# Attention and two MLPs on one core: another order of the first loads, and weights split up to two tiles sooner

## The chip, the cores and the metric

The kernel runs on one core of a Trainium2 chip. Its engines are TensorE (PE; PEld is its weight load), VectorE (DVE), ScalarE (ACT), GpSimd (POOL) and SyncE (SP), which here issues all the transfers; the core's 16 DMA engines carry them. The metric is the device time of one execution in microseconds (us); lower is better.

## The reference, cut to what matters

```python
def _attn_ref(q, k, v):                      # 2 x 8 heads, 768 positions, head size 64
    k_sum = k.reshape(B, H, nb, 32, D).max(axis=3)       # one summary key per block of 32
    v_sum = v.reshape(B, H, nb, 32, D).mean(axis=3)
    scores_l = scale * q @ k^T, kept where |i - j| < 16
    scores_s = scale * q @ k_sum^T + log(32)
    a = softmax(concat(scores_l, scores_s))
    return a @ concat(v, v_sum)

def _moe_ref(x, w_in, w_out, alpha):         # 1536 tokens, 512 -> 2048 -> 512
    h = x @ w_in
    return (max(h, 0) + alpha * min(h, 0)) @ w_out

def _moe2_ref(x, w_in, w_out, a, b):
    h = x @ w_in
    P = a[0] + a[1]*h + a[2]*h*h + a[3]*h*h*h
    Q = 1 + |b[0]|*|h| + |b[1]|*h*h
    return (P / (Q + 1e-6)) @ w_out

reference: _moe2_ref(_moe_ref(_attn_ref(q, k, v)))
```

All of it is float32.

## The kernel before

The 1536 tokens are cut into four chunks of 384 (two per batch entry). Attention is cut into 16 jobs: a job is one chunk and one pair of heads, and a chunk's four jobs give the four 128-row tiles of its `x`. Jobs 0 to 3 (the first chunk) run alone at the start; the jobs of each later chunk are woven into the steps of the first MLP on the chunk ahead of it. An MLP step (`i`, with chunk `c` and tile `f`) takes one of 16 tiles of 128 hidden columns: `hidden1(i)` is 12 matmuls into a bank `hid`, the activation is done on DVE (L810, L812), and `output1(i)` is 12 matmuls into the four banks `acc`, two steps later. The second MLP follows in the same manner with `hidden2` and `output2`.

The stages of a job are KQ (transposes of keys and queries), KX (transposes of the other keys), SC (scores, their maxima on DVE and exponentials on ACT), NM (probabilities, DVE), TR (transposes of the probabilities; ACT copies them into `pt`), AV and SU (block means of the values), and PV (probabilities times values; ACT and DVE split the result into `x_hi` and `x_lo`). Products are made of three matmuls with high and low parts, so every weight tile is split before use: ACT writes `w_in_hi` and `w_out_hi` (`w_in_high`, `w_out_high`, both through the copy at L541), POOL subtracts them from the raw tile to get `w_in_lo` (L505) and `w_out_lo` (L510). Raw weights come two tiles at a time: `load_w_in(0, n)` and `load_w_out(0, n)` bring tiles 2n and 2n+1, and `load_w(0, n)` does both.

Every engine goes through its own list in order, and waits on semaphores. For the first chunk the lists of PE, ACT and DVE are written out by hand (`FIRST_PE`, `FIRST_ACT`, `FIRST_DVE`, L69 to L78). In `FIRST_ACT` the split of `w_in` tile 0 stands ahead of (2, TR), (3, SC), (1, PV), (3, SU) and (3, TR). In `FIRST_PE` (3, AV) stands ahead of (1, PV), (2, PV) and (3, TR), and the first products `hidden1(0)` behind (3, TR). (3, AV) waits for the sums that POOL makes (L472) of the values that `first_rest(3)` loads.

In the loop over steps ACT does at each step, in this order: the attention stages that belong to the step, then `weights(0, f + 3)` (both splits of one tile, L663 to L667), then `g1_high(i)`, the high part of the activated tile, whose low part DVE makes (`g1_low`, L787). `hidden1(i)` waits for the low part of step i-2, whose bank it takes. Job 4 has its KQ at step 0, SC at step 2, TR at the start and PV at the end of step 3; job 5 has its KQ at step 4.

SP's list is the order of the loads (L370 to L416). It has waits of its own: `load_keys(j)` for j > 4 waits until PE has done the key transposes of job j-1 (`pe_k`), since `k_raw` has a single buffer, and then for the query transposes (`pe_q`); in `load_values` the copies at L342 wait for `pool_v0`. While SP waits, nothing behind it in its list is issued.

Of the kernel before, what the change touches and what calls it, by code (L numbers as in the profile page):

```python
# [13 lines left out]
def attention_two_mlps(nc, q, k, v, w_in1, w_out1, alpha, w_in2, w_out2, a_coef, b_coef, out):  # L14
# [17 lines left out]
    KD, FT = DM // P, DF // P  # L32
# [123 lines left out]
    with ExitStack() as ctx:  # L156
# [53 lines left out]
        def half(j):  # L210
            return chunk(j) % 2

        def batch(j):
            return chunk(j) // 2

        def pair(j):
            return j % NPAIR
# [13 lines left out]
        def kx_jobs(j):  # L231

            return sum(1 for n in range(j + 1) if half(n) == 0)

        def heads(p):

            return slice(2 * p, 2 * p + 2)
# [12 lines left out]
        def vgroup(j):  # L250
            return pair(j) // 2
# [12 lines left out]
        def _(sp):  # L264
            def load_pair(dst, rows, src, loaded):

                for h in range(2):
                    sp.dma_start(dst[0:rows, :, h, :], src[h].rearrange("(t p) d -> p t d", p=rows)).then_inc(loaded, 16)  # L268

            def first_k(p):  # L270
                hs = heads(p)
                load_pair(k_raw0[:, :, hs, :], KROWS[0], k[0, hs, 0:4 * KROWS[0], :], k0_loaded[p])

            def first_q(p):
                hs = heads(p)
                load_pair(q_raw0[:, :, hs, :], P, q[0, hs, 0:CH, :], q0_loaded[p])

            def first_kx(p):
                hs = heads(p)
                load_pair(kx_raw0[:, :, hs, :], KXROWS, k[0, hs, 4 * KROWS[0]:S, :], kx0_loaded[p])  # L280

            def load_keys(j):
                b, hs, n = batch(j), heads(pair(j)), KROWS[half(j)]
                s0 = 0 if half(j) == 0 else CH - WINDOW
                if j > NPAIR:
                    sp.wait_ge(pe_k, j)
                load_pair(k_raw, n, k[b, hs, s0:s0 + 4 * n, :], k_loaded)
                if j > NPAIR:
                    sp.wait_ge(pe_q, j)
                load_pair(q_raw, P, q[b, hs, half(j) * CH:half(j) * CH + CH, :], q_loaded)  # L290
                if half(j) == 0:
                    if kx_jobs(j) > NPAIR + 1:
                        sp.wait_ge(pe_kx, kx_jobs(j) - 1)
                    load_pair(kx_raw, KXROWS, k[b, hs, 4 * KROWS[0]:S, :], kx_loaded)
# [3 lines left out]
            def edge(half):  # L298

                n = KW - WINDOW  # L300
                if half == 0:
                    return 0, slice(WINDOW, KW), slice(0, n), slice(0, WINDOW)
                return UNITS - 1, slice(0, n), slice(S - n, S), slice(n, KW)

            def windows_of(b, h, half):

                rows = v[b, h]
                first = QT - WINDOW if half == 0 else CH - WINDOW
                return bass.AP(rows.tensor, rows.offset + first * D, [[D, KW], [QT * D, UNITS - 1], [1, D]])

            def first_edges():
                t, rows, inside, outside = edge(0)
                sp.dma_start(vw0[rows, t, :, :], v[0, :, inside, :].rearrange("h p d -> p h d")).then_inc(edges0_loaded, 16)
                sp.dma_start(vw0[outside, t, :, :], v[0, :, 0:WINDOW, :].rearrange("h p d -> p h d")).then_inc(edges0_loaded, 16)

            def first_rest(p):
                hs = heads(p)
                sp.dma_start(v_all[p][0:RP, :, :], v[0, hs, :, :].rearrange("h (p t) d -> p h (t d)", t=RT)).then_inc(rest0_loaded[p], 16)

            def first_windows(p):  # L320
                for h in range(2 * p, 2 * p + 2):
                    sp.dma_start(vw0[0:KW, 1:UNITS, h, :], windows_of(0, h, 0)).then_inc(v0_loaded[p], 16)

            def load_values(j):
                b, h0, s = batch(j), 2 * pair(j), j % 2
                if j >= NPAIR + 2:
                    sp.wait_ge(pe_v, j - 1)
                t0, t1 = (1, UNITS) if half(j) == 0 else (0, UNITS - 1)
                for h in range(2):
                    sp.dma_start(vw[0:KW, s, t0:t1, h, :], windows_of(b, h0 + h, half(j))).then_inc(v_loaded[s], 16)  # L330
                t, rows, inside, outside = edge(half(j))
                sp.dma_start(vw[rows, s, t, :, :], v[b, h0:h0 + 2, inside, :].rearrange("h p d -> p h d")).then_inc(v_loaded[s], 16)
                sp.dma_start(vw[outside, s, t, :, :], v[b, h0:h0 + 2, 0:WINDOW, :].rearrange("h p d -> p h d")).then_inc(v_loaded[s], 16)
                if batch(j) == 0:
                    sp.wait_ge(pool_v0, 1)
                else:
                    sp.wait_ge(pool_vs, vgroup(j) + 1)
                for h in range(2):
                    r = (pair(j) % 2) * 2 * NB + h * NB
                    rows = vsum0[:, pair(j), h, :] if batch(j) == 0 else vsum[r:r + NB, vgroup(j), :]  # L340
                    src = rows.unsqueeze(1).broadcast_to([NB, UNITS, D])
                    sp.dma_start(vw[KW:KU, s, :, h, :], src).then_inc(v_loaded[s], 16)  # L342
# [9 lines left out]
            def load_w_in(m, n):  # L352

                if m:
                    sp.wait_ge(pe_h, LAST + WG * (n + 1))
                for f in range(WG * n, WG * (n + 1)):
                    sp.dma_start(w_in_raw[:, f, :, :], w_in_v[m][:, f, :, :]).then_inc(w_in_loaded[n], 16)

            def load_w_out(m, n):

                if m:
                    sp.wait_ge(pe_o, LAST + WG * (n + 1))
                fs = slice(WG * n, WG * (n + 1))
                sp.dma_start(w_out_raw[:, fs, :], w_out_v[m][:, fs, :]).then_inc(w_out_loaded[n], 16)

            def load_w(m, n):
                load_w_in(m, n)
                load_w_out(m, n)
# [3 lines left out]
            first_kx(0)  # L372
            first_k(1)
            first_q(1)
            first_kx(1)
            first_rest(0)
            first_k(2)
            first_q(2)
            first_kx(2)
            first_rest(1)  # L380
            first_k(3)
            first_q(3)
            first_rest(2)
            first_kx(3)
            first_windows(0)
            first_edges()
            first_rest(3)
            first_windows(1)
            sp.dma_start(alpha_rows[0:FT, :], alpha.rearrange("(f p) -> f p", p=P)).then_inc(alpha_loaded, 16)
            load_w_in(0, 0)  # L390
            first_windows(2)
            first_windows(3)
            load_w_out(0, 0)
# [1 line left out]
            load_keys(4)  # L395
            load_w_out(0, 1)
            load_w(0, 2)
            load_w(0, 3)
            load_values(4)
            load_w(0, 4)  # L400
            load_keys(5)
            load_w(0, 5)
            load_values(5)
            load_w(0, 6)
# [134 lines left out]
        def _(act):  # L539
# [55 lines left out]
            def w_in_high(m, f):  # L595
                act.wait_ge(w_in_loaded[f // WG], 16 * WG * (m + 1))
                if m == 0 and f == 3:
                    act.wait_ge(pool_v0, 1)
                copy(w_in_hi[f][:, :, :].rearrange("p k c -> p (k c)"), w_in_raw[:, f, :, :].rearrange("p k c -> p (k c)")).then_inc(act_w_in, 1)
# [5 lines left out]
            def weights(m, f):  # L605
                w_in_high(m, f)
                w_out_high(m, f)
# [41 lines left out]
            for i in range(STEPS):  # L649
                c, f = i // FT, i % FT  # L650
                if i == FT + FT // 2:
                    act.wait_ge(consts_loaded, 32)
                    act.activation(ab[:, 4:6], ab[:, 4:6], ACT.Abs).then_inc(act_ab, 1)
                    act.wait_ge(act_ab, 1)
                slot(c + 1, f, 0)
                if i < R1:
                    g1_high(i)
                if i >= FT and f == LAG1 - 1:
                    chunk_done(c - 1, (0, 1))
                slot(c + 1, f, 1)  # L660
                if i >= FT and f == LAG1 - 1:
                    chunk_done(c - 1, (2, 3))
                slot(c + 1, f, 2)  # L663
                if c == 0:

                    if f + 3 < FT:
                        weights(0, f + 3)  # L667
                if i >= LAST + LW:
                    weights(1, i - LAST - LW)
                if i >= R1:  # L670
                    act.wait_ge(pe_o, i - R1 + 1)
                    g1_high(i)
# [8 lines left out]
            for i in range(STEPS + 2):  # L681
                n, f = i // FT, i % FT
# [404 lines left out]
```

## Time and profile before

| | |
|---|---|
| Median of 3 runs | 622.32 us (622.29 to 622.75) |
| The profiled execution's own time | 622.29 us |
| Its span in the profile | 620.6 us, so 1.7 us lie outside the span |
| PE busy over the span | 605.1 us, 98% |
| ACT, DVE, POOL busy over the span | 312.0, 414.3, 197.1 us |
| Share of PE in the chain that ended last | 93% |

The page gives busy time, which hides where an engine of 98% has its other 2%. So the rows below are of the first 60 us for the most part, where PE and the DMA engines change places as the one that the others wait for. Starts are us from the span's start. In a row of the timeline, what stands in brackets is how long the engine had been idle ahead of the instruction and what released it; a duration of a merged row covers all of its instructions. The granted clock of TensorE (PEclk) is 1.00 at full speed.

### The profile page before, as it was taken

Reading aid. Unit: us, or ns where it says so; the run is one execution under the profiler, and the core shown is the slowest. Engines: PE = TensorE matmul, PEld = TensorE weight load, DVE = VectorE, ACT = ScalarE, POOL = GpSimd, SP = SyncE. Lnnn points to the kernel's source line nnn. Section 1 sums busy time; section 2 is a strip of 40 time slices with the busy share of each in tenths; the row PEclk is TensorE's granted clock in tenths of the full one; section 3 lists DMA queues with packets and bytes.
Section 4 is the critical chain, followed back from the end, with each engine's and each line's share of the span. In section 5 each row is a group of like instructions: output and inputs, shape, how many; then the busy total and the mean of one; then the engine's idle time right before and its main releaser. Section 6 shows DMA issues by size and latency. Waiting matters only on the chain.

```text
span 620.6 us, 10573 instructions
## 1 busy us (share of the span) xinstructions
PE 605.1 (98%) x3897; PEld 563.5 (91%) x3897; DVE 414.3 (67%) x953; ACT 312.0 (50%) x778; POOL 197.1 (32%) x221
## 2 busy tenths in 40 slices
PE   5799999999999999999999999999999999999997
PEld 4689999999999999999999899899899899999996
DVE  4665555555654555455555699778978788778775
ACT  4784644333332433232434587657755765656564
POOL 4564559000000000000333375334434434433431
PEclk9899999999999999999999999999999999999999
DMA  8999606311222022001344300001000000001001
GB/s 181 225 265 262 165 7 132 68 28 36 64 51 45 6 50 51 2 1 62 110 135 137 102 1 1 1 0 53 1 1 1 34 18 1 0 2 51 1 2 51
DMA packets 79539, 37.30 MB, mean 60 GB/s; under 512 B 56496, under 2 KB 72896, under 8 KB 79296
## 3 DMA queue, kind: packets, MB, share of 16 engines
q1 hardware_dynamic: 79488, 36.63, 23.2%
q8 instruction: 31, 0.51, 0.3%
q14 instruction: 20, 0.16, 0.1%
HBM read 32.58 MB, written 3.15 MB: 58 GB/s over the span
## 4 chain that ended last, share of the span: by engine, by line
PE 93%; SPq 3%; DVE 1%; DMA 1%; issue 1%; ACT 0%
PE acc L947 15%; PE acc L949 14%; PE acc L948 14%; PE hid L947 11%; PE hid L949 11%; PE hid L948 11%; PE att L947 4%; PE att L949 4%; PE att L948 4%; SPq L268 2%; PE att L937 2%; PE att L874 2%; PE att L909 2%; PE att L916 1%; DMA w_in_raw<-in_moe_w_in_dram 1%
## 5 line engine op out<-in xcount | busy, mean ns | idle before, releaser
L947 PE MATMUL hid<-x_hi,w_in_hi 128*128 128x384 f32 x384 | 130.2, 339 | 0.0
L949 PE MATMUL hid<-x_hi,w_in_lo 128*128 128x384 f32 x384 | 129.1, 336 | 0.0
L948 PE MATMUL hid<-x_lo,w_in_hi 128*128 128x384 f32 x384 | 128.9, 336 | 0.0
L510 POOL TENSOR_TENSOR w_out_lo<-w_out_raw,w_out_hi 128x512 fp32r<-128x512 f32 x32 | 41.3, 1294 | 219.4 <-ACT w_out_hi L541 219.2
L947 PE MATMUL acc<-g_hi,w_out_hi 128*128 128x384 f32 x256 | 91.1, 356 | 0.0
L531 POOL TENSOR_SCALAR qpart<-habs,ab 128x384 f32<-128x384 f32 x64 | 44.0, 688 | 143.1 <-ACT poly L689 142.5
L949 PE MATMUL acc<-g_hi,w_out_lo 128*128 128x384 f32 x256 | 86.8, 339 | 0.0
L948 PE MATMUL acc<-g_lo,w_out_hi 128*128 128x384 f32 x256 | 86.5, 338 | 0.0
L541 ACT ACTIVATE g_hi<-hid 128x384 fp32r<-128x384 f32 x96 | 48.4, 504 | 67.8 <-PE acc L949 59.9
L787 DVE TENSOR_TENSOR g_lo<-hid,g_hi 128x384 fp32r<-128x384 f32 x64 | 35.6, 556 | 65.2 <-ACT g_hi L541 65.2
L949 PE MATMUL acc<-w_out_hi,g_lo 128*128 128x512 f32 x192 | 76.1, 396 | 0.0
L948 PE MATMUL acc<-w_out_lo,g_hi 128*128 128x512 f32 x192 | 75.6, 394 | 0.0
L947 PE MATMUL acc<-w_out_hi,g_hi 128*128 128x512 f32 x192 | 75.5, 393 | 0.0
L947 PEld LDWEIGHTS hid<-x_hi,w_in_hi 128*128 128x128 f32 x384 | 72.1, 188 | 1.8 <-DVE x_lo L771 0.4
L948 PEld LDWEIGHTS hid<-x_lo,w_in_hi 128*128 128x128 f32 x384 | 72.1, 188 | 1.3
L949 PEld LDWEIGHTS hid<-x_hi,w_in_lo 128*128 128x128 f32 x384 | 72.0, 188 | 0.0
L810 DVE TENSOR_SCALAR g_neg<-hid,prelu_alpha 128x384 f32<-128x384 f32 x64 | 39.4, 615 | 45.5 <-PE hid L949 45.5
L533 POOL TENSOR_TENSOR qpart<-qpart,habs 128x384 f32<-128x384 f32 x64 | 65.7, 1026 | 5.3
L947 PEld LDWEIGHTS acc<-g_hi,w_out_hi 128*128 128x128 f32 x256 | 48.0, 188 | 2.6 <-issue 1.7
L948 PEld LDWEIGHTS acc<-g_lo,w_out_hi 128*128 128x128 f32 x256 | 48.2, 188 | 0.0
L949 PEld LDWEIGHTS acc<-g_hi,w_out_lo 128*128 128x128 f32 x256 | 48.1, 188 | 0.0
L571 ACT ACTIVATE att<-att,nmax 128x120 f32<-128x120 f32 x78 | 24.7, 367 | 45.8 <-DVE nmax L755 45.8
(155 smaller groups left out, 1145.0 us busy)
## 6 DMA issues: line engine op xcount, KB each, us to landing
w_in_raw<-in_moe_w_in_dram SPq DMA_DIRECT2D x32, 256.0 KB, 4.2
w_out_raw<-in_moe_w_out_dram SPq DMA_DIRECT2D x16, 512.0 KB, 4.2
vw<-in_v_dram SPq DMA_DIRECT2D x32, 120.0 KB, 4.9
q_raw<-in_q_dram SPq DMA_DIRECT2D x32, 96.0 KB, 2.8
out_dram<-out_sb SPq DMA_DIRECT2D x12, 256.0 KB, 2.0
k_raw<-in_k_dram SPq DMA_DIRECT2D x16, 104.0 KB
k_raw<-in_k_dram SPq DMA_DIRECT2D x16, 100.0 KB
vs_raw<-in_v_dram SPq DMA_DIRECT2D x2, 768.0 KB, 7.6
```

The lines of the kernel that those rows point to most:

```text
L268: sp.dma_start(dst[0:rows, :, h, :], src[h].rearrange("(t p) d -> p t d", p=rows)).then_inc(loaded, 16)
L510: pool.tensor_tensor(w_out_lo[:, f, :], w_out_raw[:, f, :], w_out_hi[f][:, :].bitcast(F32), ALU.subtract).then_inc(pool_w_out, 1)
L531: pool.tensor_scalar(qpart[:, i % 2, :], habs[:, i % 2, :], ab[:, 5:6], ab[:, 4:5], ALU.mult, ALU.add).then_inc(pool_qb, 1)
L533: pool.tensor_tensor(qpart[:, i % 2, :], qpart[:, i % 2, :], habs[:, i % 2, :], ALU.mult).then_inc(pool_q, 1)
L541: return act.activation(dst, src, ACT.Identity)
L571: last = act.activation(scores_of(bk, h, n), scores_of(bk, h, n), ACT.Exp, scale=-1.0, bias=nmax[:, s, i:i + 1], accum_out=sums_of(bk, h)[ ...
L787: dve.tensor_tensor(g1_lo[:, i % R1, :], hid[i % 2][:, 0:CH], g1_hi[:, i % R1, :].bitcast(F32), ALU.subtract).then_inc(dve_g, 1)
L810: dve.tensor_scalar(g_neg[:, :], hb, 0.0, prelu_alpha[:, f:f + 1], ALU.min, ALU.mult).then_inc(dve_m, 1)
L874: tr = pe.transpose(dst[:, t * rows:(t + 1) * rows], rows_of_pair.rearrange("p h d -> p (h d)"), ident[0:rows, 0:rows])
L947: pe.matmul(dst, lhs[0], rhs[0], start=start, stop=False)
L948: pe.matmul(dst, lhs[0], rhs[1], start=False, stop=False)
L949: return pe.matmul(dst, lhs[1], rhs[0], start=False, stop=stop)
```

## The change

Three things are moved; no instruction is added or removed, and no size changes.

1. In the loads ahead of the loop over jobs: `first_rest(0)` ahead of `first_kx(1)`, `first_kx(2)` behind `first_k(3)`, `first_kx(3)` behind the first windows and edges of the values, and `load_w_in(0, 0)` ahead of `first_windows(1)` and of the load of `alpha_rows`.
2. `load_keys(5)` and `load_values(4)` stand ahead of `load_w(0, 3)`; before, `load_values(4)` stood behind it and `load_keys(5)` behind `load_w(0, 4)`.
3. ACT splits tiles f+3 at steps 0 and 1, then two tiles a step at steps 2 and 3 (5 and 6, 7 and 8), and tile f+5 from step 4 on.

```diff
@@ SP's list
             first_q(1)
+            first_rest(0)
             first_kx(1)
-            first_rest(0)
             first_k(2)
             first_q(2)
-            first_kx(2)
             first_rest(1)
             first_k(3)
+            first_kx(2)
             first_q(3)
             first_rest(2)
-            first_kx(3)
             first_windows(0)
             first_edges()
+            first_kx(3)
             first_rest(3)
+            load_w_in(0, 0)
             first_windows(1)
             sp.dma_start(alpha_rows[0:FT, :], alpha.rearrange("(f p) -> f p", p=P)).then_inc(alpha_loaded, 16)
-            load_w_in(0, 0)
...
             load_w(0, 2)
+            load_keys(5)
+            load_values(4)
             load_w(0, 3)
-            load_values(4)
             load_w(0, 4)
-            load_keys(5)
@@ ACT's loop over steps
-                    if f + 3 < FT:
-                        weights(0, f + 3)
+                    for n in (f + 3,) if f < 2 else (2 * f + 1, 2 * f + 2) if f < 4 else (f + 5,):
+                        if n < FT:
+                            weights(0, n)
```

SP around the first load of weights, before: `vw_49` (L322, L313, L314) are the windows and edges of the first chunk's values, `v_all_late` the values of `first_rest(3)`.

```order
L268 DMA kx_raw_70<-in_k_dram 88x4x64 x2
L322 DMA vw_49<-in_v_dram 96x5x64 x2
L313 DMA vw_49<-in_v_dram 80x8x64
L314 DMA vw_49<-in_v_dram 16x8x64
L318 DMA v_all_late<-in_v_dram 96x2x512
L322 DMA vw_49<-in_v_dram 96x5x64 x2
L389 DMA alpha_rows<-in_moe_alpha_dram 16x128
L357 DMA w_in_raw<-in_moe_w_in_dram 128x4x128 x2
```

The same place of SP's list now:

```order
L322 DMA vw_49<-in_v_dram 96x5x64 x2
L313 DMA vw_49<-in_v_dram 80x8x64
L314 DMA vw_49<-in_v_dram 16x8x64
L268 DMA kx_raw_70<-in_k_dram 88x4x64 x2
L318 DMA v_all_late<-in_v_dram 96x2x512
L357 DMA w_in_raw<-in_moe_w_in_dram 128x4x128 x2
L322 DMA vw_49<-in_v_dram 96x5x64 x2
L390 DMA alpha_rows<-in_moe_alpha_dram 16x128
```

The load of weight tiles 0 and 1 has gone ahead of three transfers, and the two of `kx_raw_70` (`first_kx(3)`) behind four.

SP from the weights of `load_w(0, 2)` on, as a difference; `k_raw` and `q_raw` are `load_keys(5)`, `vw` with L330 to L342 is `load_values(4)`.

```order
 L357 DMA w_in_raw<-in_moe_w_in_dram 128x4x128 x2
 L364 DMA w_out_raw<-in_moe_w_out_dram 128x2x512
-L357 DMA w_in_raw<-in_moe_w_in_dram 128x4x128 x2
-L364 DMA w_out_raw<-in_moe_w_out_dram 128x2x512
+L268 DMA k_raw<-in_k_dram 100x4x64 x2
+L268 DMA q_raw<-in_q_dram 128x3x64 x2
 L330 DMA vw<-in_v_dram 96x5x64 x2
 L332 DMA vw<-in_v_dram 80x2x64
```

Behind the first pair, which is `load_w(0, 2)`, the weights of tiles 6 and 7 stood next; now the keys and queries of job 5 do, then the values of job 4, and only then those weights.

ACT at steps 2 and 3, before, from the splits of tile 6 on: `pt_110` is the copy that job 4's PV reads, `g1_hi_116` the high part of a step's activation.

```order
L541 ACTIVATE g1_hi_116<-hid0 128x384
L541 ACTIVATE pt_110<-att0 120x384
L541 ACTIVATE pt_110<-att1 120x384
L541 ACTIVATE x_hi_90<-att0 128x384
L541 ACTIVATE w_in_hi6_57<-w_in_raw_67 128x512
L541 ACTIVATE w_out_hi6_78<-w_out_raw_88 128x512
L541 ACTIVATE g1_hi_116<-hid1 128x384
```

And now:

```order
L541 ACTIVATE w_in_hi6_57<-w_in_raw_67 128x512
L541 ACTIVATE w_out_hi6_78<-w_out_raw_88 128x512
L541 ACTIVATE g1_hi_116<-hid0 128x384
L541 ACTIVATE pt_110<-att0 120x384
L541 ACTIVATE pt_110<-att1 120x384
L541 ACTIVATE x_hi_90<-att0 128x384
L541 ACTIVATE w_in_hi7_58<-w_in_raw_67 128x512
L541 ACTIVATE w_out_hi7_79<-w_out_raw_88 128x512
L541 ACTIVATE w_in_hi8_59<-w_in_raw_67 128x512
L541 ACTIVATE w_out_hi8_80<-w_out_raw_88 128x512
L541 ACTIVATE g1_hi_116<-hid1 128x384
```

The splits of tile 6 have gone ahead of the high part of step 2 and of job 4's `pt`; those of tile 8 have come to step 3.

## Rows read from the trace of the kernel before

**Rows 1.** Windows: us, busy us of each engine, granted clock, DMA share, GB/s.

```profile
30.00:40.00 10.00, 8.28 (x86) 7.11 (x86) 5.35 (x15) 8.42 (x27) 5.33 (x5) 1.00 0.96 285
40.00:50.00 10.00, 10.00 (x79) 9.27 (x77) 7.46 (x26) 7.65 (x25) 7.64 (x7) 1.00 0.97 251
60.00:280.00 220.00, 220.00 (x1719) 211.32 (x1712) 122.11 (x360) 79.80 (x264) 33.60 (x30) 1.00 0.23 51
300.00:600.00 300.00, 298.62 (x1532) 275.52 (x1531) 234.42 (x420) 178.73 (x365) 122.84 (x137) 1.00 0.10 32
```

**Rows 2.** Chain that ended last, 20 to 42 us: start, us, what.

```profile
21.89 7.03 DMA w_in_raw<-in_moe_w_in_dram
...
29.60 0.87 ACT pt L541 x2
...
32.76 0.54 DVE probs L767
...
33.34 0.54 PE acc L916 x3
```

**Rows 3.** Timeline of SP, issues of transfers: start, us, instruction.

```profile
19.57 0.99 SPq L322 DMA_DIRECT2D vw<-in_v_dram  x2
20.60 0.49 SPq L389 DMA_DIRECT2D alpha_rows<-in_moe_alpha_dram  x1
21.13 1.79 SPq L357 DMA_DIRECT2D w_in_raw<-in_moe_w_in_dram  x2
...
34.36 0.51 SPq L364 DMA_DIRECT2D w_out_raw<-in_moe_w_out_dram  x1
```

**Rows 4.** Timeline of POOL and of PE, end of the first chunk's attention.

```profile
25.43 2.60 POOL L472 TENSOR_TENSOR v_all_late<-v_all_late 96x512 f32<-96x512 f32 x3 [3.73 <-DMA v_all_late<-in_v_dram]
...
28.79 0.92 PE L937 MATMUL hid<-pt,vw 120*64 120x64 f32 x24
30.61 0.92 PE L937 MATMUL acc<-pt,vw 120*64 120x64 f32 x24 [0.91 <-ACT pt L541]
```

**Rows 5.** Windows at the two clocks, same columns as rows 1.

```profile
11.70:15.10 3.40, 2.20 (x9) 1.66 (x9) 3.04 (x12) 2.61 (x13) 2.44 (x3) 1.00 0.98 218
22.00:25.30 3.30, 1.65 (x30) 1.42 (x30) 2.06 (x10) 3.25 (x15) 0.00 (x0) 1.00 1.14 232
25.40:28.70 3.30, 3.30 (x33) 2.70 (x32) 3.03 (x17) 0.80 (x1) 2.44 (x3) 0.50 0.93 170
```

**Rows 6.** Timeline of PE, one stage at either clock, and the step's start.

```profile
15.21 1.48 PE L909 MATMUL hid<-kt,qt 64*64 64x120 f32 x24
...
19.33 0.85 PE L909 MATMUL acc<-kt,qt 64*64 64x120 f32 x24
...
25.41 1.48 PE L909 MATMUL acc<-kt,qt 64*64 64x120 f32 x24
...
39.40 0.51 PE L874 MATMUL att<-ident,k_raw 100*128 100x100 f32 x4
...
50.50 0.92 PE L937 MATMUL att<-pt,vw 120*64 120x64 f32 x24
```

**Rows 7.** Timeline of SP: keys, then values with little else in the queues.

```profile
46.52 0.87 SPq L268 DMA_DIRECT2D k_raw<-in_k_dram  x2
47.44 0.95 SPq L268 DMA_DIRECT2D q_raw<-in_q_dram  x2
...
98.39 0.96 SPq L330 DMA_DIRECT2D vw<-in_v_dram  x2
...
100.42 1.68 SPq L342 DMA_DIRECT2D vw<-kx_raw  x2
102.14 1.05 SPq L268 DMA_DIRECT2D k_raw<-in_k_dram  x2
...
292.58 1.02 SPq L357 DMA_DIRECT2D w_in_raw<-in_moe_w_in_dram  x2
```

**Rows 8.** L364, issue to landing, in three places: at 292.2, 46.0 and 56.0 us.

```profile
DMA to landing us min/median/max: 3.5/3.5/3.5
...
DMA to landing us min/median/max: 4.0/4.0/4.0
...
DMA to landing us min/median/max: 6.2/6.2/6.2
```

**Rows 9.** Timeline of ACT, splits of tile 5 up to job 4's `pt`.

```profile
47.22 0.72 ACT L541 ACTIVATE w_out_hi<-w_out_raw 128x512 fp32r<-128x512 f32 x1
47.74 0.58 ACT L541 ACTIVATE g_hi<-hid 128x384 fp32r<-128x384 f32 x1
48.11 0.98 ACT L541 ACTIVATE pt<-att 120x384 f32<-120x384 f32 x2
```

**Rows 10.** Waits of PE from 130 us on: for whom, us, times, longest.

```profile
PE att L947 <- DVE g_lo L825: 1.4, 1, 1.4
```

## The prediction, made before the changed kernel was run

> **What bounds the kernel now.** I read four views, in this order. The windows come first: PE is busy for 8.28 of the 10 us from 30 to 40, and for all of the time from 40 on, with 300 to 600 us short by the 1.4 us of one wait [rows 1, 10]. So from about 40 us on a microsecond saved on another engine is worth nothing, and a microsecond of PE's waiting costs a full one. The same rows show the DMA engines at 0.96 and 0.97 of their time up to 50 us: the start of the kernel is bound by what arrives when, the rest by PE. Second, the chain of waits between 20 and 42 us: it goes over the transfer of weight tiles 0 and 1 (7.03 us), the split of tile 0 on ACT behind it, then `pt` of job 2 at 29.60, the exponentials and probabilities of job 3, and PE's transposes of them at 33.34, behind which the first products stand [rows 2]. Third and fourth, the timelines of SP, PE, POOL and ACT around the places that the change touches.
>
> The sum is made against the profiled execution, 622.29 us (span 620.6 and 1.7 outside it); the median of the runs is 622.32, the same to 0.03. A measurement of this kernel can tell about 0.2%, 1.24 us, from no change.
>
> **The loads at the start.** In SP's list the weights of tiles 0 and 1 pass the windows of pair 1 and `alpha_rows`. The issue began at 21.13; what it passes began at 19.57, so it begins 1.56 us sooner [rows 3]. The DMA engines are full there (1.14 of a stretch of 3.30 us, 22.0 to 25.3) [rows 5], so what counts is the work that is passed, and it is of the same size as its issue. I take 1.45 us, between 1.0 and 1.6. The other moves (`first_rest(0)` with `first_kx(1)`, `first_kx(2)`, `first_kx(3)`) change places among transfers that all stand ahead of the weights, so they move PE's early work by up to 1 us to and fro, but not the landing of the weights. What PE gains there it doesn't keep: (3, AV) waits for POOL's sums, which begin at 25.43 when `first_rest(3)` has landed and take 2.60 [rows 4], and as many bytes stand ahead of `first_rest(3)` as before. So (1, PV) stays at 28.8. It also needs the windows of pair 1, which now land behind the weights, at about 28.9 - 0.3; I take them as just in time (cost 0 to 0.5).
>
> Behind (1, PV) the gain is real: ACT gets to `pt` of job 2 1.45 us sooner, so (2, PV), which waited 0.91 us for it at 30.61 [rows 4], and the transposes of job 3, which waited for the probabilities, move with it. All that follows up to KQ of job 4 at 39.40 [rows 6] is a row of waits on this chain: **minus 1.45 us**.
>
> **The clock at that place.** SC of one job took 0.85 us at 19.33 and 1.48 at 25.41, in the stretch in which the granted clock was 0.50, TensorE's level of 1.2 GHz instead of 2.4 [rows 5, 6]. It had fallen when PE had worked 1.65 of 3.30 us, and came back after PE had worked without a break (3.30 of 3.30). With the change PE does its scores and transposes of jobs 2 and 3 up to 1 us sooner and then has nothing to do until POOL's sums at 28.0, so it works less from 25.4 to 28.7, and I take it that the clock comes back one such stretch later. Work for 2.20 of 3.40 us from 11.7 on did not bring it up: the scores at 15.21 still took 1.48 us (the view prints 1.00 there, but the duration is that of the low clock) [rows 5, 6]. Then (1, PV) and (2, PV), 0.92 us each, run at the low clock; by the scores' 1.48 to 0.85 each takes some 0.65 more, and as half of the first hides in ACT's work, **plus 0.7 us**, from 0 (clock is up) to 1.3. KQ of job 4 then begins at 39.40 - 1.45 + 0.7 = 38.65.
>
> **The keys of job 5 ahead of tiles 6 and 7.** This is the edit that costs. `load_keys(5)` waits for KQ of job 4. Before, it came up at 46.52 [rows 7], long after KQ, and waited for nothing. Now SP comes to it when the issue of `load_w(0, 2)` ends, at 34.87 [rows 3], and stands until 38.65 + 0.51 plus 0.04. Behind it in the queue stand `load_values(4)`, `load_w(0, 3)` and all that follows. I count in the times of before, where KQ ends at 39.91, and put the shift of -0.75 in at the end. Keys from 39.95, 0.92; queries 0.99 (both with the gap to the next row); the values 3.76 (98.39 to 102.14); `w_in` of tiles 6 and 7 1.05 [rows 7]; so the issue of their `w_out` begins at 46.7. From issue to landing it took 3.5 us in a quiet stretch, 4.0 behind values and `w_in` as here, 6.2 at 56 us with full queues [rows 8]. The backlog has run down meanwhile, so I take 4.0, the nearest place: 50.7, with 50.2 and 52.9 as bounds.
>
> Who waits for that: at step 2 ACT now splits tiles 5 and 6, and behind tile 6 stand `g1_high(2)` and job 4's `pt`. From the begin of a `w_out` split to the end of both copies of `pt` it takes 47.22 to 49.09, 1.87 us [rows 9]. So `pt` is done at 52.6, and PV of job 4 on PE, which began at 50.50 [rows 6], begins at 52.6: **plus 2.1 us**, with 1.6 and 4.3 as bounds. `hidden1(4)`, which needs the low part of step 2, stands behind PV and finds it ready. The extra split itself (two of some 0.52 us) is hidden behind the landing. At step 3 ACT splits tiles 7 and 8; `load_w(0, 4)` is issued right behind `load_w(0, 3)`, and PV of job 4 stands between on PE and ACT, so I take 0, with 0.5 as bound. From step 4 on one tile a step is split two steps sooner than before; PE never waited for a tile there, so gain 0. SP's next wait, in `load_keys(6)`, is on job 5 at step 4, which is done by the time that SP comes to it, as before.
>
> **The sum.** -1.45 + 0.7 + 2.1 = +1.35: 622.29 + 1.35 = **623.6 us**. The gain of the start is there, and the queue behind a waiting load takes it back.
>
> **What a page says of the landing.** The Trainium skill (DMA: Bandwidth & Descriptors, Anatomy of one DMA) fits a transfer as about 2.0 us and its bytes at 436 GB/s, measured for transfers of GpSimd. For 512 KB that is an estimate of 3.2 us; the rows above have 3.5 at the least, and with 3.2 the sum would be 622.8.
>
> **The rivals.**
> (a) The clock is up again at (1, PV), as before. For it: how PE works from 25.4 to 28.7 depends on some tenths; before it was up. Then -1.45 + 2.1 = +0.65: 622.9.
> (b) The weights land as in the quiet row, 3.5: +0.85, 623.1. For it: SP stood for nearly 4 us and the queues ran down. Against it: values and `w_in` stand just ahead.
> (c) The clock falls because of the new wait. PE stands for about 2.1 us before PV of job 4. At 1.2 GHz half of a stretch like that of rows 5 is lost, 3.3 / 2 = 1.65 us: 625.3. For it: it fell to 0.50 at 25.4 after waits that together were shorter. Against it: the work was light there and is dense here, and the one wait of 1.4 us later left it at 1.00 [rows 1, 10].
> (d) The queues are as full as at 56 us, and `w_out` takes 6.2: +2.2 on the sum, 625.8.
> (e) Faster. ACT finds tiles 6 and 7 landed when it comes to them, and only the gain of the start is left: 622.29 - 1.45 = 620.8. It decides at some 48 us in the times of before: `w_out` of tiles 6 and 7 would have to be there by then. Before, ACT never waited for it; now 6.7 us of issues stand between KQ of job 4 and its own issue, so I see no way to that but much shorter issues.
>
> **How the numbers follow.** Forecast 0.32, (a) 0.25, (b) 0.09, (c) 0.18, (d) 0.11, (e) 0.05. Likeliest is 623.6. Within 0.2% (621.1 to 623.55) lie (a), (b) and about a third of the forecast's own spread (623.0 to 624.2): 0.45. Faster is (e): 0.05. Slower is the rest: 0.50. The range reaches from below (a), with a little more gain at the start, to (c): 622.1 to 625.4; outside are (e), most of (d) and a corner of (a).
>
> **What would show it.** In the changed kernel's trace: the split of tile 0 on ACT at about 27.5 instead of 28.9; (1, PV) still at 28.8, and POOL's last sums still from 25.4; the windows with the granted clock at 0.50 behind 28.8 (the term of 0.7) or not; SP's waits with one more of about 4 us on PE's key transposes (L268); ACT waiting about 3 us for `w_out_raw` or `w_in_raw` ahead of the splits of tile 6; and PE waiting about 2 us for ACT's `pt` ahead of PV of job 4. It is wrong if SP doesn't stand there, if ACT's wait for tile 6 is under 1 us, or if PE's list before 40 us has not moved by 0.5 to 1.5 us.

## The result

| | before | changed |
|---|---|---|
| Median | 622.31 us (621.32 to 622.75, 4 runs) | 626.79 us (626.60 to 627.32, 4 runs) |
| Profiled execution | 622.29 us, span 620.6 | 627.17 us, span 625.5 |
| Ratio | | 1.0084, 95% interval 1.0060 to 1.0107 |

The change makes the kernel slower: by 4.5 us or 0.72% by the medians, by 0.84% as the ratio was measured. Two more executions of the changed kernel are on record beside the four, the profiled one with 627.17 us and one with 629.26. The forecast was slower by 1.3 us with a range up to 625.4: the sign is right, the size is not. PE executes as many instructions as before, and the whole difference lies in the first 60 us. The windows of the changed kernel, to be read beside [rows 1] (us, busy us of PE, PEld, DVE, ACT and POOL, granted clock, DMA share, GB/s):

```profile
30.00:40.00 10.00, 9.07 (x112) 7.74 (x111) 5.45 (x18) 8.50 (x25) 4.34 (x5) 1.00 0.92 262
40.00:50.00 10.00, 10.00 (x79) 9.29 (x78) 6.00 (x24) 6.93 (x23) 7.62 (x7) 1.00 0.64 154
50.00:60.00 10.00, 6.78 (x53) 6.33 (x52) 3.66 (x7) 6.00 (x15) 6.06 (x6) 0.83 1.09 299
60.00:280.00 220.00, 220.00 (x1721) 211.06 (x1721) 123.19 (x362) 78.34 (x262) 32.63 (x30) 1.00 0.25 56
300.00:600.00 300.00, 298.62 (x1536) 276.06 (x1535) 233.81 (x418) 177.75 (x362) 123.57 (x136) 1.00 0.10 33
```

From 60 us on nothing has changed (from 62 to 600 us PE is busy for 536.62 us in either trace, with the granted clock at 1.00). From 50 to 60 PE is idle for 3.2 us and the granted clock is down for part of the time. From 40 to 50 the DMA engines work 0.64 of the time, where before it was 0.97: the queues run dry twice, with 0.10 from 40 to 41 and 0.21 from 45 to 47. The changed kernel's timeline of SP shows why; it ends the issue of `load_w(0, 2)` at 35.6 us and issues nothing until 40.08:

```profile
35.12 0.51 SPq L364 DMA_DIRECT2D w_out_raw<-in_moe_w_out_dram  x1
40.08 0.79 SPq L268 DMA_DIRECT2D k_raw<-in_k_dram  x2
40.91 0.94 SPq L268 DMA_DIRECT2D q_raw<-in_q_dram  x2
41.90 1.02 SPq L330 DMA_DIRECT2D vw<-in_v_dram  x2
...
43.98 1.78 SPq L342 DMA_DIRECT2D vw<-kx_raw  x2
45.80 1.07 SPq L357 DMA_DIRECT2D w_in_raw<-in_moe_w_in_dram  x2
46.91 0.51 SPq L364 DMA_DIRECT2D w_out_raw<-in_moe_w_out_dram  x1
```

The chain that ended last goes over just these issues. This is its end, from the `w_out` of tiles 6 and 7 (start, us, what):

```profile
46.91 5.09 DMA w_out_raw<-in_moe_w_out_dram
...
52.13 0.43 issue
52.56 0.47 ACT g_hi L541
53.03 0.77 ACT pt L541 x2
...
53.94 1.55 PE att L938 x24
```

And the timelines of ACT and of PE at the same place, which answer to [rows 9] and [rows 6]:

```profile
47.37 0.72 ACT L541 ACTIVATE w_out_hi<-w_out_raw 128x512 fp32r<-128x512 f32 x1
49.64 0.63 ACT L541 ACTIVATE w_in_hi<-w_in_raw 128x512 fp32r<-128x512 f32 x1 [1.55 <-DMA w_in_raw<-in_moe_w_in_dram]
52.02 0.63 ACT L541 ACTIVATE w_out_hi<-w_out_raw 128x512 fp32r<-128x512 f32 x1 [1.75 <-DMA w_out_raw<-in_moe_w_out_dram]
52.56 0.47 ACT L541 ACTIVATE g_hi<-hid 128x384 fp32r<-128x384 f32 x1
52.93 0.86 ACT L541 ACTIVATE pt<-att 120x384 f32<-120x384 f32 x2
```

```profile
39.54 0.51 PE L875 MATMUL att<-ident,k_raw 100*128 100x100 f32 x4
...
53.94 1.55 PE L938 MATMUL att<-pt,vw 120*64 120x64 f32 x24 [3.22 <-ACT pt L541]
...
58.45 0.51 PE L875 MATMUL att<-ident,k_raw 100*128 100x100 f32 x4
```

ACT has split tile 5 and waits twice for tile 6; `pt` of job 4 stands behind it, and PE waits 3.22 us for `pt`. PV then takes 1.55 us instead of 0.92.

**Where the 4.9 us of span went.** KQ of job 4 begins at 39.54, before at 39.40: 0.14. From there to PV of job 4 it is 14.40 us, before 11.10: 3.30. From PV to KQ of job 5 it is 4.51 us, before 3.07 (50.50 to 53.57): 1.44, with the same instructions. That makes 4.88, the whole difference.

The last of these is TensorE's clock. In the windows of the changed kernel PE does nothing from 51.0 to 53.8, and then the granted clock is 0.50, the level of 1.2 GHz:

```profile
51.00:53.80 2.80, 0.00 (x0) 0.00 (x0) 0.74 (x2) 1.77 (x4) 1.84 (x2) 1.00 1.05 345
53.90:57.20 3.30, 3.26 (x30) 3.18 (x31) 1.37 (x3) 1.68 (x4) 0.59 (x1) 0.50 1.13 336
```

### The profile page after: what moved, and what is told of

Same layout as the page of the kernel before. It is cut to its first block, busy times and chain, and to the rows that moved or that the text cites. A ratio compares the mean times of both kernels' runs of the same rounds, so it can differ in the third digit from the quotient of the medians.

```text
span 625.5 us, 10573 instructions
## 1 busy us (share of the span) xinstructions
PE 608.0 (97%) x3897; PEld 566.8 (91%) x3897; DVE 415.2 (66%) x953; ACT 312.7 (50%) x778; POOL 196.9 (31%) x221
## 2 busy tenths in 40 slices
DMA packets 79539, 37.30 MB, mean 60 GB/s; under 512 B 56496, under 2 KB 72896, under 8 KB 79296
## 4 chain that ended last, share of the span: by engine, by line
PE 92%; SPq 3%; DMA 1%; DVE 1%; ACT 1%; issue 1%; ACTq 0%
PE acc L948 15%; PE acc L950 14%; PE acc L949 14%; PE hid L948 11%; PE hid L950 10%; PE hid L949 10%; PE att L948 4%; PE att L950 4%; PE att L949 4%; SPq L268 2%; PE att L938 2%; PE att L875 1%; PE att L910 1%; PE att L917 1%; DMA w_out_raw<-in_moe_w_out_dram 1%; DMA kx_raw<-in_k_dram 1%
## 5 line engine op out<-in xcount | busy, mean ns | idle before, releaser
L788 DVE TENSOR_TENSOR g_lo<-hid,g_hi 128x384 fp32r<-128x384 f32 x64 | 35.6, 556 | 69.3 <-ACT g_hi L541 69.3
```

What stands on the lines that cost most here:

```text
L788: dve.tensor_tensor(g1_lo[:, i % R1, :], hid[i % 2][:, 0:CH], g1_hi[:, i % R1, :].bitcast(F32), ALU.subtract).then_inc(dve_g, 1)
```

## The experiments

The theory: the loss is made by two parts together. `load_keys(5)` and its wait hold up the weights behind them, and ACT's earlier split of tile 6 makes PE need these weights four microseconds sooner. The rivals: the start's new order costs; two splits in a step are too much for ACT; the late landing costs by itself; the clock has nothing to do with it. Twelve kernels were run, each against the kernel before on the same chip. A median is of 11 or 12 executions, but of 6 in "all but the start's loads" and of 5 in "PE kept busy". The kernel before had medians of 622.31 to 622.70 us beside them, so that an expected time missed by a tenth or two says little.

| kernel | ratio to before | 95% interval | median, us |
|---|---|---|---|
| start's loads alone | 0.9993 | 0.9983 to 1.0003 | 621.91 |
| all but the start's loads | 1.0102 | 1.0081 to 1.0123 | 628.43 |
| splits alone | 0.9993 | 0.9979 to 1.0007 | 621.88 |
| queue alone | 1.0012 | 1.0002 to 1.0022 | 623.04 |
| changed, `load_w(0, 3)` first | 0.9996 | 0.9985 to 1.0007 | 622.53 |
| changed, values behind | 0.9995 | 0.9983 to 1.0007 | 622.28 |
| changed, `pt` first | 1.0001 | 0.9989 to 1.0013 | 622.25 |
| changed, PE kept busy | 1.0046 | 1.0033 to 1.0058 | 625.43 |
| start, and `w_out` tile 2 later | 0.9982 | 0.9970 to 0.9994 | 621.68 |
| `w_out` tile 2 later alone | 1.0011 | 0.9998 to 1.0024 | 622.90 |
| `w_in` sooner, `w_out` tile 2 later | 1.0003 | 0.9989 to 1.0017 | 622.76 |
| changed, values behind, `w_out` tile 2 later | 0.9993 | 0.9979 to 1.0008 | 622.29 |

### The parts one by one

The loads at the start alone; the diff is the first part of the one above.

> The kernel before with the new order of the loads at the start alone; the later loads and ACT's splits are as before. Theory (a queue behind a waiting load, with ACT's splits on top): this part is worth nothing and costs nothing, 622.0 to 622.8 us; the weights of tiles 0 and 1 land some 2 us sooner, but PE's transposes of job 2 at the low clock take the place of the wait. Rival (the start itself costs): up to 626.8 us.

0.9993: no difference that can be told. Everything but the start:

> The changed kernel with the start's loads as before: keys(5) and values(4) ahead of load_w(0, 3), and the splits up to two tiles sooner. Theory: all of the loss is here: 626 to 627.5 us, with a wait of PE of about 3 us ahead of PV of job 4. Rival (start): 622.3 us.

1.0102, more than the whole change, and 0.9 us above the expected range; PE's wait was 4.2 us and not about 3. The mechanism is the same, only later: `w_out` of tile 6 is there at 53.5, PE waits for `pt`, and the clock falls after it. So the loss is all in the queue and the splits. (By the ratios the start's order makes the whole change some 1.1 us less slow; the two intervals overlap, so that isn't shown.)

The splits alone:

```diff
-                    if f + 3 < FT:
-                        weights(0, f + 3)
+                    for n in (f + 3,) if f < 2 else (2 * f + 1, 2 * f + 2) if f < 4 else (f + 5,):
+                        if n < FT:
+                            weights(0, n)
```

> The kernel before with ACT's splits up to two tiles sooner alone. Theory: tiles 6 and 7 have landed at 45.1 us before ACT comes to them at 47.9, so ACT doesn't wait; pt of job 4 is done 1.0 us later, at 50.1, and PV of job 4 on PE comes at 50.5: 622.3 us, within 0.3. Rival (two splits in a step are too much for ACT): PE waits 1 to 3 us, 623.5 to 626 us.

0.9993. ACT does both tiles without a wait, and its `pt` is done in time (timeline of ACT):

```profile
46.48 0.72 ACT L541 ACTIVATE w_in_hi<-w_in_raw 128x512 fp32r<-128x512 f32 x1
47.00 0.72 ACT L541 ACTIVATE w_out_hi<-w_out_raw 128x512 fp32r<-128x512 f32 x1
47.52 0.58 ACT L541 ACTIVATE g_hi<-hid 128x384 fp32r<-128x384 f32 x1
47.90 0.97 ACT L541 ACTIVATE pt<-att 120x384 f32<-120x384 f32 x2
```

PV of job 4 began at 49.24 in that execution, 0.4 us behind the end of `pt`. Two splits in a step are not too much. The queue alone:

```diff
             load_w(0, 2)
+            load_keys(5)
+            load_values(4)
             load_w(0, 3)
-            load_values(4)
             load_w(0, 4)
-            load_keys(5)
```

> The kernel before with keys(5) and values(4) ahead of load_w(0, 3) alone; ACT splits one tile a step. Theory: the weights of tiles 6 and 7 land at 52 us as in the changed kernel, but ACT comes to tile 6 at 51.9 and not at 47.9, behind pt and PV of job 4, and g1_high(3) has over 2 us to spare: 622.3 us, within 0.3. Rival (the late landing costs by itself, whoever splits when): 624 to 626 us.

1.0012, 0.7 us in the medians, where nothing was expected: close to nothing, though the interval just leaves 1 out. SP stands as in the changed kernel and the weights come as late, but ACT comes to tile 6 only behind PV of job 4 (timelines of SP and of ACT):

```profile
35.54 0.51 SPq L364 DMA_DIRECT2D w_out_raw<-in_moe_w_out_dram  x1
39.60 0.79 SPq L268 DMA_DIRECT2D k_raw<-in_k_dram  x2
...
51.17 0.49 ACT L541 ACTIVATE x_hi<-att 128x384 fp32r<-128x384 f32 x1 [2.41 <-PE att L937]
51.55 0.62 ACT L541 ACTIVATE w_in_hi<-w_in_raw 128x512 fp32r<-128x512 f32 x1
52.08 0.62 ACT L541 ACTIVATE w_out_hi<-w_out_raw 128x512 fp32r<-128x512 f32 x1
```

By the medians neither part alone costs 1 us (the queue's interval reaches to 1.4); both together cost 4.5 to 6.1. Here the late queue did little harm as long as its reader came late too.

### The changed kernel with one link cut

The next three leave the start and the two-tile splits as changed, and each cuts one link. First the queue: `load_w(0, 3)` goes ahead of the wait.

```diff
             load_w(0, 2)
+            load_w(0, 3)
             load_keys(5)
             load_values(4)
-            load_w(0, 3)
             load_w(0, 4)
```

> The changed kernel with load_w(0, 3) back ahead of load_keys(5) and load_values(4); the start's loads and ACT's splits stay changed. Theory: nothing that ACT needs at step 2 stands behind SP's wait any more, so the loss of 4.5 us is gone: 621.5 to 622.5 us, perhaps a few tenths under the kernel before. Rival (start and splits together cost): 624 us or more.

0.9996: the loss is gone. Then only what stands between the wait and the weights:

```diff
             load_keys(5)
-            load_values(4)
             load_w(0, 3)
+            load_values(4)
             load_w(0, 4)
```

> The changed kernel with load_values(4) behind load_w(0, 3); load_keys(5) with its wait stays ahead of it. It takes 3.8 us of issues out from between SP's wait and the weights. Theory: w_out of tiles 6 and 7 lands near 48.5 us instead of 52.0, PE's wait of 3.2 us shrinks to under 0.5, and TensorE's clock stays up: 622.0 to 623.0 us. Rival (the wait of SP alone does it, how much stands behind it doesn't matter): 625 us or more.

0.9995. SP still stands for its wait (2.1 us here, as KQ of job 4 came at 37.91 and `load_w(0, 2)` was issued by 36.31) and then needs only the keys' issues ahead of the weights (timelines of SP and of ACT):

```profile
38.45 0.79 SPq L268 DMA_DIRECT2D k_raw<-in_k_dram  x2
39.28 0.94 SPq L268 DMA_DIRECT2D q_raw<-in_q_dram  x2
40.27 1.03 SPq L357 DMA_DIRECT2D w_in_raw<-in_moe_w_in_dram  x2
41.35 0.51 SPq L364 DMA_DIRECT2D w_out_raw<-in_moe_w_out_dram  x1
...
48.03 0.72 ACT L541 ACTIVATE w_out_hi<-w_out_raw 128x512 fp32r<-128x512 f32 x1
48.55 0.58 ACT L541 ACTIVATE g_hi<-hid 128x384 fp32r<-128x384 f32 x1
48.92 0.97 ACT L541 ACTIVATE pt<-att 120x384 f32<-120x384 f32 x2
```

So it isn't the wait as such but the wait and the 3.9 us of issues behind it (41.90 to 45.80 in the changed kernel). It was close: the landing took 6.6 us, so `w_out` was there at 47.95, and ACT came to it at 48.03. Third, the link on ACT: tile 6 is split behind job 4's `pt`.

```diff
                 slot(c + 1, f, 0)
+                if i == 3:
+                    weights(0, 6)
...
-                    for n in (f + 3,) if f < 2 else (2 * f + 1, 2 * f + 2) if f < 4 else (f + 5,):
+                    for n in (f + 3,) if f < 3 else (2 * f + 1, 2 * f + 2) if f < 4 else (f + 5,):
```

> The changed kernel with the splits of tile 6 moved on ACT from step 2 to behind the two copies of pt of job 4 at step 3; the loads stay as changed. Theory: the weights still land near 52 us and ACT still waits for them, but pt, which PV of job 4 needs, stands ahead of that wait, so PE doesn't wait: 621.7 to 623.0 us. Rival (the late landing costs wherever ACT waits for it): 625 us or more.

1.0001. ACT waits for the late weights as in the changed kernel, but nobody waits for ACT (timeline of ACT):

```profile
47.20 0.87 ACT L541 ACTIVATE pt<-att 120x384 f32<-120x384 f32 x2
48.50 0.63 ACT L541 ACTIVATE w_in_hi<-w_in_raw 128x512 fp32r<-128x512 f32 x1 [0.43 <-DMA w_in_raw<-in_moe_w_in_dram]
51.09 0.63 ACT L541 ACTIVATE w_out_hi<-w_out_raw 128x512 fp32r<-128x512 f32 x1 [1.95 <-DMA w_out_raw<-in_moe_w_out_dram]
```

### The clock

PE gets work to do during its wait: zeros are added to a sum that is open anyway. The loads and splits are those of the changed kernel. `NIDLE` is 14, and POOL fills `zeros` at the start.

```diff
                 elif stage == PV:
+                    if j == NPAIR:
+                        for _ in range(NIDLE):
+                            pe.matmul(acc[3][:, 0:P], ident[:, :], zeros[:, :], start=False, stop=False)
```

> The changed kernel with 14 matmuls of zeros, added to a sum that is open anyway, ahead of PE's wait for pt of job 4: it gives PE some 1.7 to 3 us of work in a wait of 3.2 us. Theory (1.4 us of the loss is TensorE's clock, which fell to 0.50 after that wait): the clock stays at 1.00 and PV and hidden1(4) take 0.9 and 2.2 us instead of 1.55 and 3.0: 625.0 to 625.6 us. Rival (the clock had nothing to do with the wait): 626.8 us, or more if the matmuls reach beyond the wait.

1.0046, 625.43 us: 1.4 us less than the changed kernel by the medians (2.4 by the ratios, each against before on its own chip, whose intervals, 1.0033 to 1.0058 and 1.0060 to 1.0107, do not overlap), though `pt` came later in the profiled execution (PV at 54.58, not 53.94). The timeline of PE and the windows:

```profile
50.48 3.29 PE L932 MATMUL acc<-zeros,ident 128*128 128x128 f32 x28
...
54.58 0.92 PE L944 MATMUL att<-pt,vw 120*64 120x64 f32 x24 [0.82 <-ACT pt L544]
...
57.62 0.51 PE L878 MATMUL att<-ident,k_raw 100*128 100x100 f32 x4
```

```profile
50.40:53.80 3.40, 3.36 (x30) 3.17 (x28) 0.09 (x1) 1.17 (x4) 2.49 (x2) 1.00 1.06 341
53.90:57.20 3.30, 2.62 (x34) 2.58 (x35) 2.01 (x4) 2.20 (x6) 0.58 (x1) 1.00 1.13 331
```

The clock stays at 1.00, PV takes 0.92 us, and from PV to KQ of job 5 it is 3.04 us, as before the change (3.07) and not 4.51. So the clock fell because PE stood idle in that wait, and the fall cost 1.4 us. The Trainium skill (TensorE: Matmul & The Clock Gate, Part 1: The HAM clock gate (the "warmup" mystery)) says that activity keeps the clock up and idleness lets it fall; these rows agree.

### Where the gain of the start went

In the traces with the start changed and no wait later on, KQ of job 4 began at 38.42, 37.80, 37.91 and 37.74 (start alone, weights first, values behind, `pt` first), 1.0 to 1.7 us ahead of the 39.40 of before. Part of that is chance. In the five traces with the old start it began between 38.14 and 40.02, 39.06 on average, and in the eight with the whole new start between 37.74 and 39.54, 38.36 on average: 0.7 us sooner, with a spread within each order of about 1.8 us. The times hardly show it. One reason may be a wait behind it. This is ACT in the trace of the changed kernel with the values behind, then PE:

```profile
35.03 1.14 ACT L541 ACTIVATE w_out_hi<-w_out_raw 128x512 fp32r<-128x512 f32 x2
38.59 0.63 ACT L541 ACTIVATE w_out_hi<-w_out_raw 128x512 fp32r<-128x512 f32 x1 [2.42 <-DMA w_out_raw<-in_moe_w_out_dram]
39.13 0.47 ACT L541 ACTIVATE g_hi<-hid 128x384 fp32r<-128x384 f32 x1
...
40.34 0.41 PE L948 MATMUL hid<-x_hi,w_in_hi 128*128 128x384 f32 x1 [1.58 <-DVE g_lo L788]
```

The split of `w_out` tile 2, which nobody needs before step 4, waits for its weights, and `g1_high(0)` stands behind it, for which PE waits ahead of `hidden1(2)`. The same wait of PE is 0.79 us with the weights first and 0.73 with `pt` first, but there is none in the trace of the start alone, so that it can't be all of the reason. Moving that split behind KQ of job 4 should let the gain through:

```diff
-                 (2, WI), (0, WO), (1, WO), (2, WO)]
+                 (2, WI), (0, WO), (1, WO)]
...
                 if c == 0:
+                    if f == 0:
+                        w_out_high(0, 2)
```

> The kernel before with the new order of the loads at the start, and ACT's split of w_out tile 2 moved from ahead of g1_high(0) to behind KQ of job 4. Theory: the gain of the start (KQ of job 4 some 1 to 1.5 us sooner) is capped because g1_high(0) stands behind a split that waits until w_out of tiles 2 and 3 lands near 37.5 to 38.5 us, and hidden1(2) needs the low part of step 0; with the split out of the way 620.8 to 621.6 us. Rival (the gain isn't there, low clock and transfers eat it): as with the start alone, 621.9 to 622.3 us.

0.9982, interval 0.9970 to 0.9994: 621.68 us against 622.70 on the same chip. It is the only kernel here whose interval lies under 1, one of twelve, and it overlaps with that of the start alone (0.9983 to 1.0003); the time is just outside the expected 620.8 to 621.6. `g1_high(0)` is at 37.30 in its trace and PE doesn't wait for it. Two controls, that edit alone, and it with only the weights of tiles 0 and 1 brought forward:

> The kernel before with ACT's split of w_out tile 2 behind KQ of job 4 alone. Theory: in the trace of before g1_high(0) waited for DVE and not for the split, so there is nothing to gain in most executions: 622.0 to 622.4 us. Rival (the split's place matters by itself): 621.5 us or less.

> The kernel before with load_w_in(0, 0) ahead of first_windows(1) and alpha_rows alone, the keys and rest loads as before, and the split of w_out tile 2 behind KQ of job 4. Theory: the one move that brings the weights sooner is enough, and the early keys of pairs 2 and 3, which come sooner in this order, keep PE ahead: 620.6 to 621.4 us, at or under the kernel with the whole new start. Rival (the other moves of the start are what gains): 622.0 us or more.

1.0011 and 1.0003. The first is as expected, or a trifle slower. The second missed: I had thought the one move of the weights enough. Its trace has PE waiting 2.9 us for the windows of the values ahead of PV of job 0, and (3, AV) at 29.16 instead of 28.15; PE's list of transposes was late, not the weights. In the five traces with the wholly old start PE waited 0.8 to 3.4 us there, in the eight with the whole new one at most 0.2. That speaks for the keys' place behind the values' windows as part of the gain; by the times it isn't shown, as the intervals of this kernel and of the one with the whole new start touch (0.9989 and 0.9994). Last, the edit on the changed kernel with the values behind:

> The changed kernel with load_values(4) behind load_w(0, 3), and besides it ACT's split of w_out tile 2 behind KQ of job 4. With the values behind alone, the trace showed PE waiting 1.6 us for the low part of step 0 ahead of hidden1(2), since g1_high(0) stood behind that split. Theory: that wait goes and the time is 621.0 to 621.9 us, some 0.1 to 0.2% under the kernel before. Rival (the wait only moves to the next stage): 622.2 us or more.

0.9993, 622.29 us: not told apart from before or from its base, and a miss, with the time of the rival. The wait for the low part of step 0 is gone from its trace, but in this execution the granted clock was low when PV of jobs 1 and 2 ran, and KQ of job 4 came at 38.65 instead of 37.91 (timeline of PE):

```profile
28.91 1.55 PE L940 MATMUL hid<-pt,vw 120*64 120x64 f32 x24
30.24 1.49 PE L940 MATMUL acc<-pt,vw 120*64 120x64 f32 x24
...
38.65 0.51 PE L877 MATMUL att<-ident,k_raw 100*128 100x100 f32 x4
```

Whether this split holds the gain back in general stays open: the one kernel gains without it in the way, the other can't be told.

## Why the prediction was right in sign and wrong in size

The mechanism that was to cost (SP's wait, the late weights, ACT's split ahead of `pt`, PE's wait) is the one that the experiments show. The step that failed is in the sum: it left the clock's fall after the new wait at nothing, as a rival of 0.18, and that fall cost 1.44 us. Two of its terms were mis-sized besides: the delay of PV of job 4 was 3.30 us and not 2.1, mostly by the landing, and the start gave +0.14 and not -0.75. From the forecast's 623.64 that is 1.44 + 1.20 + 0.89 more, 627.17 us, the time of the profiled execution.

- **SP's wait.** As predicted: one wait more, 4.5 us long, and the issue of the weights 7.37 us behind the begin of KQ of job 4 (46.91 to 39.54); I had counted 7.3.
- **The landing.** This term was mis-sized. I took 4.0 us, with 6.2 as bound; it was 5.1. In the four other traces in which SP stood and the values came ahead of these weights it took 5.6, 5.5, 5.1 and 4.9. I had argued that the backlog had run down and that the transfer would be quick. The queues were as good as dry just ahead of it (0.21 from 45 to 47 us), and it was slow all the same; behind it SP issued the next weights at once. Whether those took its share is not tested. The row of 4.0 was also one draw: the same transfer (tiles 8 and 9 with keys behind it, as before the change) took 5.9, 5.5, 4.0, 5.0 and 3.8 in five other traces with that order.
- **ACT and PE.** As predicted: `g1_high(2)` and `pt` behind tile 6, 1.9 us from the split to PV. The delay of PV, with the landing, is 3.30 us instead of 2.1.
- **The clock after the wait** was rival (c), with 0.18 and 1.65 us. It came, and cost 1.44. A wait of 2.1 us was longer than the 1.4 us after which the clock had not fallen, and the longer landing made it 3.2. The price of the clock and the length of the wait hang together, and I had treated them as separate cases; the range didn't hold both at once. In the trace with a 4.2 us wait the clock fell as well. No trace has a wait of about 2 us in dense work, so whether the forecast's own wait would have brought it down stays open.
- **The start.** -1.45 for the weights and +0.7 for the clock were forecast, -0.75 together; it was +0.14 in the profiled execution. The weights were there by 28.08 at the latest, but the clock came up later (the six transposes of job 1 still took 1.53 us at 21.61), and the transposes of job 2 ran low at 28.55 (1.53 us), so that ACT waited 0.78 us for them and not for the weights. The step that failed here is that PE's early work would come up to 1 us sooner and (1, PV) stay at 28.8: the scores of job 3 came at 27.14, before at 25.41, and (1, PV) at 30.23. The term of +0.7 for two PVs at the low clock was not there (0.92 us each at most). Nor is it typical: over whole executions the median of the mean granted clock is 0.997 to 1.000 in five kernels with the new start and without the wait of 3 us, 0.996 in a sixth (values behind, `w_out` tile 2 later), and 0.994 to 0.995 in the kernel before beside them; by these records the clock falls less with the new order, not more. The average of the traces above, 0.7 us sooner for KQ of job 4, is near the forecast's 0.75, but not by its two terms. The idea that (3, AV) holds on to POOL's sums was right where PE was quick (it waited for them and began at 28.12 to 28.19 in five traces, at 28.64 in a sixth), not here, where PE came to it at 29.88.
- **What was costed at nothing** held: the splits alone, the split at step 3, the later waits of SP.

## What to carry to other kernels

Before a load is moved ahead of others, look at what it waits for: everything behind it in that queue inherits the wait and the issues between. Then look at which in-order engine reads the delayed data and what stands behind that reader; moving the reader sooner and the data later each cost little or nothing alone here. And when a new wait of the matrix engine may grow past those after which your traces show the clock still up, add the clock to its price, in the same case and not in another.

## What the runs showed of the hardware

- The granted clock fell after a wait of 3.2 us and cost 1.44 us on top, and after one of 4.2 us, where PV to KQ of job 5 took 4.57 us (3.07 before); 3.3 us of matmuls of zeros during the wait kept it up. After the wait of 1.4 us at the change from the first MLP to the second it stayed up in every trace.
- When the clock first comes up differs from execution to execution of like kernels: the scores of job 2 took 0.85 us at 19.33 before and 1.48 us at 20.20 in the changed kernel. So the stage ahead of the first products is longer or shorter. Single executions of one kernel spread over 2 to 5 us; in the kernel before, those with a mean granted clock of 0.997 or more took 0.3 to 1.8 us less on each of the four chips than those with 0.992 or less, so the clock can be a part of that spread, not all of it.
- A 512 KB transfer issued into queues that had just run dry, with more weights issued behind it, took 4.9 to 5.6 us in five traces. With the queues busier (0.43 to 1.14 of the 2 us ahead, against 0.17 to 0.25) and keys issued behind it, it took 3.8 to 5.9 us in six (4.0 in [rows 8]); and 6.6 us at 41.35 in the kernel with the values behind, where the DMA engines had worked 0.94 of the 2 us ahead of it. An idle queue at the issue did not make it quick.
